# A mixture-of-experts block behind linear attention: gate logits carried with the values, and expert rows gathered through a table

## The chip, the core and the metric

The kernel runs on one core of a Trainium2 chip. The metric is the device time of one execution in microseconds (us); lower is better. The core has five engines that work side by side and meet at semaphores: TensorE (PE; its weight loads are shown apart as PEld), VectorE (DVE), ScalarE (ACT), GpSimd (POOL) and SyncE (SP), which here only issues transfers.

## What is computed

Three blocks in a row, all in float32: a decaying linear attention over 2 sequences of 768 tokens with 8 heads of 48, a mixture of 8 experts with one expert per token, and a dense block.

```python
for t in range(S):                                  # attention, per batch and head
    cur = einsum('bhd,bhe->bhde', u[None] * kt, vt)
    y[:, :, t] = einsum('bhd,bhde->bhe', rt, state + cur)
    state = w[None, :, :, None] * state + einsum('bhd,bhe->bhde', kt, vt)

logits = x @ w_gate                                 # experts: x is (1536, 384), w_gate (384, 8)
expert_idx = argmax(logits, axis=1)
gate_w = softmax(logits)[arange(N), expert_idx]
for i in range(N):                                  # tokens keep their order inside an expert
    e = expert_idx[i]
    if counts[e] < capacity:                        # capacity is 384
        disp[e, counts[e]] = x[i]; pos[i] = counts[e]; counts[e] += 1; keep[i] = True
y = einsum('ecf,efd->ecd', relu(einsum('ecd,edf->ecf', disp, w1)), w2)
out[i] = gate_w[i] * y[expert_idx[i], pos[i]]       # 0 where not kept

h = x @ w_in; g = h - tanh(h); out = g @ w_out      # dense block
```

## The kernel before

**Attention.** 12 tiles ("steps", n = 0 to 11) of 128 tokens, six per sequence, all heads at once. Inside a tile the recurrence is a product of decayed keys and queries. TensorE does, in step n and in this order: the key-query products into `pA` (lines 1140, 1144); the tile's share of the next state into `pT` (1165); the old state's share of the output into `pY` (1174), which waits until the tile before has been read out of `pY`; `own_products(n + 1)`, the diagonal term u*r*k per head (1105); `x_transposed(n - 1)`, three transposes of the finished tile (1084); once VectorE has copied the lower triangle of `pA` to `At` (880), the products of `At` with the values into `pY` (1189); `own_transposed(n + 1)` (1116); `logits(n - 1)`, three products of the transposed tile with the gate weights (1094). At n = 6, the start of the second sequence, there is no old state, and so no 1174. VectorE runs `output` (859, which makes tile x), `queries` (792), the copy to `At` (880), `keys` (784) and the new state (890) in every step. ScalarE copies transposes and logits out of PSUM and scales queries and states. GpSimd multiplies `rkf` (481), `kend` (489) and `vdiag` (507). SP loads the tiles three steps ahead (`feature_part`, `token_part`, `value_part`).

**Routing.** Tiles go in groups of 4, 4, 2 and 2 (`GROUPS`). `route1(g)` finds each token's expert on VectorE from the copied logits, a chain of some ten small dependent operations; `route2(g)` finds the gate weight, the position in the expert (from two TensorE products, `positions`) and the slot. `ROUTE1` and `ROUTE2` say in which steps they run. ScalarE scales the rows of x by the gate weight (`scale_x`; `SCALED` says when). GpSimd then scatters each tile's rows to their slots in `x_by_slot` in DRAM with an indirect DMA (`scatter`, line 472; `SENT` says when); ScalarE's queue has filled that tensor with zeros before, in nine pieces (line 650). SP loads an expert's 384 slots with a plain DMA (`expert_rows`, lines 411, 412, 421, 426). The tiles 8 to 11 are late, so for expert 0 they go to TensorE directly: `spots_of` makes a one-hot matrix and `direct` (1205) places the rows, on top of the rows that were loaded (`loaded`, 1211).

**Experts.** For expert e TensorE does `first` (72 products of 224 columns, float32 as three products of high and low parts), `transposed_rows` for expert e + 1 (1254, needs its loaded rows), and `second` (72 products). The weights are streamed by SP through four raw buffers; ScalarE makes the high part (580), VectorE the low part of w1 (849), GpSimd the low part of w2 (`low`, 460, four per expert). GpSimd's order around them is written out: four `low` of expert 0, six `token_ranks` (indirect DMAs, line 521), four `low` of expert 1, six `token_ranks`, then a loop over the other experts. A raw buffer is free for the next weights once its low part is made.

**Dense block and end.** TensorE runs without a pause; the result rows are scattered by GpSimd (550).

## Time and profile before

| | |
|---|---|
| median of 3 runs | 412.27 us (409.12 to 420.2) |
| the profiled execution: time | 410.51 us |
| its span, first to last instruction | 408.8 us |
| mean granted TensorE clock | 0.98 |
| busy: PE, PEld | 384.9 us (94%), 373.1 us (91%) |
| busy: DVE, ACT, POOL | 214.2 us (52%), 180.9 us (44%), 155.7 us (38%) |
| attention: start to the last `output` | 0 to 77.5 us |
| routing tail: to expert 0's first product | 77.5 to 92.9 us |
| experts | 92.9 to 230.6 us |
| dense block and end | 230.6 to 408.8 us |

The busy shares are means over stages that differ. TensorE is close to always busy from 92.9 us on; before that, it shares the bound with others. A line of the timeline reads: start, duration, engine, line, operation, output<-inputs, shape, count, and in brackets how long the engine was idle before and what ended that. "issue" and "remote" are idle times that nothing in the kernel's own waits explains. The clock is given as a share of 2.4 GHz.

### The profile page before, as it was taken

Reading aid. Unit: us, or ns where it says so; the run is one execution under the profiler, and the core shown is the slowest. Engines: PE = TensorE matmul, PEld = TensorE weight load, DVE = VectorE, ACT = ScalarE, POOL = GpSimd, SP = SyncE. Lnnn points to the kernel's source line nnn. Section 1 sums busy time; section 2 is a strip of 40 time slices with the busy share of each in tenths; the row PEclk is TensorE's granted clock in tenths of the full one; section 3 lists DMA queues with packets and bytes.
Section 4 is the critical chain, followed back from the end, with each engine's and each line's share of the span. In section 5 each row is a group of like instructions: output and inputs, shape, how many; then the busy total and the mean of one; then the engine's idle time right before and its main releaser. Section 6 shows DMA issues by size and latency. Waiting matters only on the chain.

```text
span 408.8 us, 10468 instructions
## 1 busy us (share of the span) xinstructions
PE 384.9 (94%) x3738; PEld 373.1 (91%) x3739; DVE 214.2 (52%) x453; ACT 180.9 (44%) x486; POOL 155.7 (38%) x132
## 2 busy tenths in 40 slices
PE   7999898698999999999999899999999999999991
PEld 7777687598999999999999899999999999999991
DVE  7667978574555655555465356615252434343340
ACT  5553456434564665756656454533022313231220
POOL 3966665435877742715517051541002000110002
PEclk9999999689999999999999999999999999999997
DMA  7989986444849478576684527000000000010001
GB/s 246 271 251 269 249 211 220 141 149 154 264 162 285 150 249 261 189 253 192 224 284 158 182 79 226 6 21 38 0 0 19 38 0 0 0 58 0 0 0 65
DMA packets 41541, 56.85 MB, mean 139 GB/s; under 512 B 3584, under 2 KB 39104, under 8 KB 41504
## 3 DMA queue, kind: packets, MB, share of 16 engines
q1 hardware_dynamic: 35936, 46.23, 36.9%
q10 hardware_dynamic: 3600, 5.31, 4.1%
q0 software_dynamic: 1968, 4.83, 3.1%
q8 instruction: 22, 0.36, 0.4%
q14 instruction: 15, 0.12, 0.1%
HBM read 46.23 MB, written 10.13 MB: 138 GB/s over the span
## 4 chain that ended last, share of the span: by engine, by line
PE 58%; issue 18%; POOL 13%; DVE 4%; DMA 2%; ACT 2%; another core or an unknown queue 1%; POOLq 0%; DVEq 0%; SPq 0%; ACTq 0%
POOL w_lo L460 11%; PE ring L1065 9%; PE ring L1067 9%; PE ring L1066 9%; PE pO L1317 8%; PE pO L1316 8%; PE pY L1189 2%; POOL token_of_rank L521 2%; PE ring L1205 2%; PE pA L1140 2%; PE pD L1094 1%; DVE At L880 1%; PE pY L1174 1%; PE pX L1084 1%
## 5 line engine op out<-in xcount | busy, mean ns | idle before, releaser
L460 POOL TENSOR_TENSOR w_lo<-raw_weights,w_hi 128x768 fp32r<-128x768 f32 x40 | 73.5, 1846 | 84.6 <-ACT w_hi L580 84.3
L1007 DVE SCALAR_TENSOR_TENSOR minus_tanh<-square,ring 128x384 f32<-128x384 f32 x64 | 35.5, 554 | 93.5 <-ACT square L730 79.1
L580 ACT ACTIVATE w_hi<-raw_weights 128x768 fp32r<-128x768 f32 x80 | 67.1, 848 | 28.5 <-DMA raw_weights<-w 28.4
L730 ACT ACTIVATE square<-ring 128x384 f32<-128x384 f32 x64 | 31.4, 491 | 94.7 <-DVE h_hi L1017 53.8
L1065 PE MATMUL ring<-yT_hi,w_hi 128*128 x192 | 65.0, 339 | 1.7 <-DVEq L1002 1.7
L1316 PE MATMUL pO<-w_hi,h_hi 128*128 128x384 f32 x192 | 64.9, 338 | 0.0
L1317 PE MATMUL pO<-w_lo,h_hi 128*128 128x384 f32 x192 | 64.8, 338 | 0.0
L1066 PE MATMUL ring<-yT_lo,w_hi 128*128 x192 | 64.8, 338 | 0.0
L1067 PE MATMUL ring<-yT_hi,w_lo 128*128 x192 | 64.8, 338 | 0.0
L1065 PE MATMUL ring<-xT_hi,w_hi 128*128 128x224 f32 x192 | 52.9, 275 | 1.6 <-issue 1.1
L849 DVE TENSOR_TENSOR w_lo<-raw_weights,w_hi 128x768 fp32r<-128x768 f32 x40 | 42.4, 1073 | 22.3 <-ACT w_hi L580 18.7
L550 POOL DMA_INDIRECT out<-out_rows,tok x12 | 11.7, 976 | 111.1 <-ACT out_rows L725 107.2
L1065 PE MATMUL pO<-h_hi,w_hi 128*128 128x224 f32 x192 | 53.2, 277 | 0.0
L1067 PE MATMUL ring<-xT_hi,w_lo 128*128 128x224 f32 x192 | 52.6, 274 | 0.6 <-issue 0.6
L1066 PE MATMUL ring<-xT_lo,w_hi 128*128 128x224 f32 x192 | 52.6, 274 | 0.0
L1067 PE MATMUL pO<-h_hi,w_lo 128*128 128x224 f32 x192 | 52.6, 274 | 0.0
L1066 PE MATMUL pO<-h_lo,w_hi 128*128 128x224 f32 x192 | 52.6, 274 | 0.0
L967 DVE SCALAR_TENSOR_TENSOR h_lo<-ring,h_hi 128x224 fp32r<-128x224 f32 x64 | 24.3, 390 | 32.9 <-ACT h_hi L697 30.9
L1065 PEld LDWEIGHTS ring<-xT_hi,w_hi 128*128 128x128 f32 x192 | 36.8, 192 | 2.8 <-issue 2.0
L1065 PEld LDWEIGHTS ring<-yT_hi,w_hi 128*128 128x128 f32 x192 | 36.0, 188 | 1.9 <-issue 1.9
L1065 PEld LDWEIGHTS pO<-h_hi,w_hi 128*128 128x128 f32 x192 | 36.8, 192 | 0.1
L1067 PEld LDWEIGHTS pO<-h_hi,w_lo 128*128 128x128 f32 x192 | 36.9, 192 | 0.0
(158 smaller groups left out, 744.1 us busy)
## 6 DMA issues: line engine op xcount, KB each, us to landing
raw_weights<-w SPq DMA_DIRECT2D x80, 384.0 KB
x_by_slot<-x ACTq DMA_DIRECT2D x9, 576.0 KB, 4.4
x_expert<-x_by_slot SPq DMA_DIRECT2D x8, 576.0 KB
kv<-kv_by_token SPq DMA_DIRECT2D x22, 192.0 KB, 4.2
rkT<-rk_by_feature SPq DMA_DIRECT2D x18, 192.0 KB, 5.1
rkT<-rk_by_feature SPq DMA_DIRECT2D x3, 512.0 KB, 4.5
x_expert<-x_by_slot SPq DMA_DIRECT2D x1, 384.0 KB
x_by_slot<-x,sloti POOLq DMA_INDIRECT x12, 4.1
```

The lines of the kernel that those rows point to most:

```text
L460: pool.tensor_tensor(lo, unit_raw(2, k), hi.bitcast(F32), ALU.subtract).then_inc(w2_ready, 1)
L550: pool.indirect_dma_start(out=out_d, out_offset=bass.IndirectOffsetOnAxis(ap=tok3[:, i:i + 1], axis=0), in_=ost[:, i, :], in_offset=None). ...
L580: act.activation(hi, unit_raw(what, k), ACT.Copy).then_inc(w1_hi if what == 1 else w2_hi, 1)
L730: act.activation(sq[:, i % 2, :], ring[i % 4][:, 0:CAP], ACT.Square, scale=THIRD ** 0.5, accum_out=sqsum[:, bass.ds(t * (2 * FC) + i, 1)]) ...
L849: dve.tensor_tensor(lo, unit_raw(1, k), hi.bitcast(F32), ALU.subtract).then_inc(w1_ready, 1)
L967: dve.scalar_tensor_tensor(out=hl[:, f, 0:cols], in0=ring[f % 4][:, 0:cols], scalar=0.0, in1=hh[:, f, 0:cols].bitcast(F32), op0=ALU.max, o ...
L1007: dve.scalar_tensor_tensor(out=nt[:, i % 2, :], in0=sq[:, i % 2, :], scalar=1.0, in1=ring[i % 4][:, 0:CAP], op0=ALU.subtract, op1=ALU.mult ...
L1065: pe.matmul(out, hi, m_hi, start=first, stop=False)
L1066: pe.matmul(out, hi, m_lo, start=False, stop=False)
L1067: return pe.matmul(out, lo, m_hi, start=False, stop=last)
L1316: pe.matmul(pO[k][:, 0:D], g, W2h[:, s, f, :], start=starts, stop=False)
L1317: last = pe.matmul(pO[k][:, 0:D], g, W2l[:, s, f, :], start=False, stop=(ends and not general))
```

## The change

- **Logits ride with the values.** A head's values get eight more columns (`DV = DH + E` = 56, tile `vg`), that hold v times the gate weights of that head. They come out of `own_products`, which now also multiplies the values by feature (a third plane of the tile `rkT`, so SP loads half as much again there) with the gate weights, and out of the transpose behind it; ScalarE copies them into `vg` (`gated_values`). All products with values or states are 56 columns wide instead of 48. The logits are then a sum over the heads of columns of x: one more `tensor_reduce` in `route1`. `x_transposed`, `xt_copy`, `logits` and `logit_copy` go.
- **Rows are stored by token.** SP stores tile n to `x_by_token` with a plain DMA once it is scaled. The zero fill and the scatters go.
- **Experts gather.** A table says which row each slot holds: `places_of` (five small VectorE operations per group, two of them new to the chain) and `spread` (two `tensor_scalar` per tile on GpSimd, 128x24 and 128x128) make one-hot tiles, `tabled` multiplies them on TensorE (8 tiles, later 4), `table_copy` reads them out on ScalarE. GpSimd then gathers an expert's three blocks of 128 rows with three indirect DMAs (`gather`), at the place in its own queue that the new loop gives.
- The parts of the routing run one or two steps earlier (`ROUTE1`, `ROUTE2`, `SCALED`); `low` for w1 of expert 0 is moved behind the routing on VectorE.

```diff
-ROUTE1 = {5: 0, 9: 1}
-ROUTE2 = {6: 0, 10: 1}
-SCALED = {8: [0, 1], 9: [2, 3], 11: [4, 5, 6, 7]}
-SENT = {9: [0, 1], 10: [2, 3], 11: [4, 5, 6, 7]}
+ROUTE1 = {4: 0, 8: 1, 10: 2}
+ROUTE2 = {5: 0, 9: 1}
+PLACES = {6: 0}
+SPREAD = {10: 0, 11: 1}
+SCALED = {6: [0], 7: [1], 8: [2], 9: [3], 10: [4, 5], 11: [6, 7]}
...
+            for n in range(STEPS):
+                sp.wait_ge(xg_ready, n + 1)
+                sp.dma_start(x_d[1 + n * P:1 + (n + 1) * P, :], row(n)).then_inc(stored[n], 16)
+            for k in range(4):
+                unit(2, 0, k)
...
+            def spread(g):
+
+                pool.wait_ge(places_ready, g + 1)
+                if g == 2:
+                    pool.wait_ge(table_full, 1)
+                first, m = GROUPS[g]
+                for n in range(first, first + m):
+                    pool.tensor_scalar(qhot[:, n % DIRECT, :], counts[:, :], reached[:, n:n + 1], None, ALU.is_equal)
+                    last = pool.tensor_scalar(phot[:, n % DIRECT, :], lanes[:, :], lane_no[:, n:n + 1], tokno[:, n:n + 1],
+                                              ALU.is_equal, ALU.mult)
+                last.then_inc(hot_ready, 1)
...
+            def expert_rows(e):
+
+                pool.tensor_copy(row3[:, :], row_i[:, e, :]).then_inc(row3_made, 1)
+                pool.wait_ge(row3_made, e)
+                for k in range(BLOCKS):
+                    gather(x_d, row3, k, xe_in)
+
+            pool.wait_ge(table_done, 1)
+            link(pool.tensor_copy(early_i[:, :], table[:, 0, 0:BLOCKS]))
+            pool.wait_ge(zero_in, 16)
+            for n in range(DIRECT):
+                pool.wait_ge(stored[n], 16)
+            gather(x_d[0:1 + DIRECT * P, :], early_i, 0, xe_in)
+            gather(x_d[0:1 + DIRECT * P, :], early_i, 1, xe_in)
+            spread(2)
+            spread(3)
+            gather(x_d[0:1 + DIRECT * P, :], early_i, 2, xe_rest_in)
+            pool.wait_ge(table_done, 2)
...
+            expert_rows(1)
...
                 for n in range(e * C, (e + 1) * C):
                     token_ranks(n)
+                pool.wait_ge(ring_full, e * RING + (RING + KD))
+                expert_rows(e + 2)
...
+            def gated_values(n):
+
+                act.wait_ge(dg_full, n + 1)
+                act.wait_ge(value_in[n % 3], 16 * (n // 3 + 1))
+                act.copy(vg[:, n % 3].rearrange("p (a b) e -> p a b e", b=2)[:, :, :, DH:DV],
...
             scale_x(10)
             scale_x(11)
+            table_copy(1)
...
+            def places_of(g, link):
+
+                first, m = GROUPS[g]
+                tiles = slice(first, first + m)
+                link(dve.tensor_tensor(allf[:, 2, tiles], allf[:, 1, tiles], limit[:, tiles], ALU.is_lt))
                 link(dve.copy_predicated(tokslot[:, tiles], allf[:, 2, tiles].bitcast(U32), allf[:, 1, tiles]))
...
+                link(dve.tensor_tensor(past[:, 0:m], bc(tokslot[:, tiles].unsqueeze(2), [P, m, Q + 1]),
+                                       bc(bounds[:, :].unsqueeze(1), [P, m, Q + 1]), ALU.is_ge))
+                link(dve.tensor_reduce(reached[:, tiles], past[:, 0:m], AX.X, ALU.add))
+                dve.scalar_tensor_tensor(out=lane_no[:, tiles], in0=reached[:, tiles], scalar=float(P),
+                                         in1=tokslot[:, tiles], op0=ALU.mult, op1=ALU.subtract).then_inc(places_ready, 1)
...
+                pe.wait_ge(feature_in[n % 3], loaded_features(n))
+                for p in range(NP):
+                    last = pe.matmul(pX[32 * p:32 * p + 2 * E + 2, D:D + P], own_gate[:, 1, p, :], rkT[:, n % 3, 2, p, :],
+                                     start=False, stop=True, skip_group_check=True)
...
+            def tabled(tiles, hot):
+
+                pe.wait_ge(hot_ready, hot)
+                for n in tiles:
+                    last = pe.matmul(pD[:, 0:Q], phot[:, n % DIRECT, :], qhot[:, n % DIRECT, :], start=(n == tiles[0]),
+                                     stop=(n == tiles[-1]))
+                last.then_inc(table_full, 1)
...
+            tabled(range(DIRECT), 2)
+            pe.wait_ge(x_ready, STEPS)
             for c in range(KD):
                 direct(8, c, near, True, False)
...
+            pe.wait_ge(table_done, 1)
+            tabled(range(DIRECT, STEPS), NG)
```

## Rows read from the trace of the kernel before

**Rows 1.** The page's slices (40 of 10.2 us): TensorE's granted clock, in tenths.

```profile
PEclk9999999689999999999999999999999999999997
```

**Rows 2.** Busy time by stretch: window, its length, PE PEld DVE ACT POOL, PEclk, DMA share, GB/s.

```profile
20.00:40.00 20.00, 18.31 (x483) 15.25 (x484) 13.12 (x20) 9.33 (x40) 12.17 (x11) 1.00 0.85 253
...
120.00:150.00 30.00, 29.77 (x267) 29.59 (x266) 17.98 (x33) 17.82 (x39) 18.36 (x13) 1.00 0.75 237
```

**Rows 3.** Chain of work that ended last, attention step 3: start, us, engine, tile, line.

```profile
25.97 0.21 PE pA L1140
...
26.99 0.60 PE pT L1165 x16
27.59 0.61 PE pY L1174 x32
28.20 0.33 PE pX L1105 x8
28.54 0.48 PE pX L1084 x3
29.01 1.07 PE pY L1189 x32
30.08 0.26 PE pX L1116
30.34 0.57 PE pD L1094 x6
30.91 0.21 PE pA L1140
```

**Rows 4.** Timeline: one 128x128 operation of GpSimd, three rows of VectorE around `route1(0)`.

```profile
1.88 0.29 POOL L444 TENSOR_SCALAR_AFFINE_SELECT before<-ones 128x128 f32<-128x128 f32 x1
...
39.49 1.07 DVE L800 TENSOR_TENSOR ldiff<-logit,lmax 128x32 f32<-128x32 f32 x1
...
41.77 0.19 DVE L808 TENSOR_TENSOR onehot<-prio,allf 128x32 f32<-128x32 f32 x1
...
43.04 0.56 DVE L859 TENSOR_TENSOR x<-vdiag,pY 128x384 f32<-128x384 f32 x1
```

**Rows 5.** Timeline, all engines: two stalls, the routing tail, expert 0's first product.

```profile
62.90 0.48 ACT L584 COPY xT<-pX 128x384 f32<-128x384 f32 x1 [3.03 <-remote]
...
77.48 0.55 DVE L859 TENSOR_TENSOR x<-vdiag,pY 128x384 f32<-128x384 f32 x1 [2.03 <-remote]
...
80.93 4.08 PE L1205 MATMUL ring<-kw,x 128*128 128x224 f32 x10
...
86.69 1.48 PE L1211 MATMUL ring<-ident,x_expert 128*128 128x128 f32 x12
...
88.00 2.46 PE L1205 MATMUL ring<-At,x 128*128 128x224 f32 x12
...
92.94 0.36 PE L1065 MATMUL ring<-xT_hi,w_hi 128*128 128x224 f32 x1 [1.14 <-issue]
```

**Rows 6.** Timeline of GpSimd and TensorE in the first experts.

```profile
105.16 1.52 POOL L521 DMA_INDIRECT token_of_rank<-tokrow,rank_i  x1
...
112.39 0.96 POOL L521 DMA_INDIRECT token_of_rank<-tokrow,rank_i  x1 [0.30 <-issue]
115.67 7.26 POOL L460 TENSOR_TENSOR w_lo<-raw_weights,w_hi 128x768 fp32r<-128x768 f32 x4 [2.32 <-ACT w_hi L580]
...
119.20 0.82 PE L1254 MATMUL ring<-ident,x_expert 128*128 128x128 f32 x6
...
136.43 0.82 PE L1254 MATMUL ring<-ident,x_expert 128*128 128x128 f32 x6
```

**Rows 7.** The page's DMA issues: out<-in, queue, count, KB each, median us to landing.

```profile
rkT<-rk_by_feature SPq DMA_DIRECT2D x3, 512.0 KB, 4.5
x_by_slot<-x,sloti POOLq DMA_INDIRECT x12, 4.1
...
out<-out_rows,tok POOLq DMA_INDIRECT x12, 2.5
```

340 lines of the change are left out of this document (161 added, 179 removed).

## The prediction

> **What bounds the kernel now.** I read the page's slices first, then the busy times by stretch, the chain of waits, and the timeline of single stretches. TensorE runs at its upper level, 2.4 GHz, in all but two slices of 10.2 us, around 71 to 92 us [rows 1]. From the first expert on it is the bound: 29.77 us busy of 30 [rows 2]. Between 20 and 40 us it is busy for 18.31 of 20 us, and the transfer engines take a share of 0.85 at 253 GB/s [rows 2]. One attention step of the chain, 4.94 us from `pA` to `pA`, has TensorE work alone in it: `pA` 1.02 (25.97 to 26.99), then 0.60, 0.61, 0.33, 0.48, 1.07, 0.26 and 0.57 [rows 3]. So a product less in a plain step is time less. This isn't so where the router runs: `route1(0)` holds VectorE from the end of its state copy to the `output` at 43.04, nearly 4 us, because some of its operations last 1.07 instead of 0.19 us beside GpSimd's [rows 4]. The routing tail, from the `output` at 77.48 to expert 0's first product at 92.94, is 15.46 us of waiting in turns [rows 5]. So the change acts at three places: the steps, the tail, and GpSimd's queue in the experts, where it adds.
>
> **Attention, part by part.** All terms are us against the profiled execution.
> - Start: the first feature load grows from 512 to 768 KB. A load of 512 KB lands after 4.5 us [rows 7], and 262 kB at 253 GB/s [rows 2] are 1.0 us; part of it hides behind the powers that VectorE makes meanwhile. Bounds 0 and +1.0, taken +0.8.
> - A plain step loses the transposes (0.48) and the logits (0.57) and gains a second set of own products (0.33) [rows 3]: -0.72. The three groups that become 56 wide (0.60 + 0.61 + 1.07 = 2.28 us) cost nothing if their count sets them, and 2.28 x 8/48 = 0.38 if the columns do. Half, +0.2, since four small products overlap in the array. So -0.5 per step, and 11 x -0.5 = -5.5 if all steps were plain. VectorE's 13.12 us and GpSimd's 12.17 us of 20 [rows 2] cover a step of 4.4 us.
> - The new copy `gated_values` goes to ScalarE behind the transpose, and `pT` waits for it. `pA` (1.02) lies between [rows 3]; the copy is a few tenths. Nothing, but 0.3 per step if ScalarE is late by that much more. Behind it in ScalarE's queue stand the diagonals, for which GpSimd's `vdiag` waits, a step ahead of need.
> - `route1(0)` moves from step 5 to 4, `route1(1)` from 9 to 8. At step 5 it stood ahead of step 6, which has no old-state products; now 1174 of the next step needs the `output` that is queued behind it. It keeps its nearly 4 us and gets a reduce of 256 elements, about 0.3 (the ones of 32 elements take 0.19 [rows 4]). TensorE has about 1.8 us of other work meanwhile (`pA`, `pT`), and the rest of 4.3 us, less the tail of the step before, is waited for: I take +1.2 for each, +2.4 together, bounds 0 and +4.
> - `places_of` is five operations, of 0.19 to 0.3 us, for each of the first two groups, less three that `route2` loses: +0.6 each, +1.2.
> - The scatters held GpSimd, and two idle times are there that no wait of the kernel explains, 3.03 us on ScalarE before 62.90 and 2.03 us on VectorE before 77.48 [rows 5]. Both stand where scatters are issued, but also where the program runs into new code. About 3 us of the last steps hang on them; the nearest bounds are 0 and -3 and nothing separates them, so -1.2.
> - The zero fill (9 x 576 KB) goes, and 3 x 64 KB of features and 32 KB of values are more per step: fewer bytes, no term.
>
> Sum to the last `output`: 0.8 - 5.5 + 2.4 + 1.2 - 1.2 = -2.3, so near 75.2.
>
> **Tail.** The logits of the last tile come 2.8 us sooner after its `output`, as neither transposes nor copies nor products precede `route1(3)`. What ends last is then another path: 16 passes of `tabled` at 0.1 us (the pace of line 1211's 12 in 1.48, less at full clock [rows 5]) 1.6; copies 0.7; the first gather's issue 1.3; the second landing 4.1 after its issue [rows 7]; `loaded` 1.5 [rows 5]; the second `tabled` 0.8; `table_copy`, which now stands in front of the splits in ScalarE's queue, 0.3, and the splits 1.1; and TensorE's restart 1.4. That is 12.8 at the upper clock. The stretch from 80.93 shows 0.41 per product at 1.2 GHz against 0.2 from 88.00 on [rows 5]; with all TensorE parts doubled it is 12.8 + 1.6 + 1.5 + 0.8 = 16.7, and 18 with `direct` late too. `spread` (two operations per tile, 0.15 and 0.29 by [rows 4]; 0.9 a pair if two scalars slow it) hides behind the last step for tiles 0 to 7, and behind the gathers for 8 to 11. I take 15.0: -0.5. Expert 0 starts at 92.94 - 2.3 - 0.5 = 90.1.
>
> **Experts.** SP's plain loads become GpSimd's. An indirect issue takes 112.39 + 0.96 - 105.16 = 8.2 us for six, or 1.37 each [rows 6]; three are 4.1 us, and the last lands 2.5 to 4.1 us after its issue began [rows 7], 1.5 to 3.1 behind its end. GpSimd's queue from expert 0's first product on: expert 1's gathers until +4.6, four `low` 7.3 [rows 6], six ranks 8.2, expert 2's gathers 4.1: done at +24.2, landed at +25.7 to +27.3. TensorE wants these rows at 119.20 - 92.94 = +26.3 [rows 5, 6]: a stall of 0 to 1.0. Then 7.3 + 8.2 + 4.1 more: done at +43.8, landed at +45.3 to +46.9; wanted at 136.43 - 92.94 = +43.5 [rows 5, 6]. Both stalls together are 1.8 to 3.4; as single issues take 1.52 [rows 6], I take 3.2. From expert 3 on the queue holds 7.3 + 4.1 = 11.4 of 16.7 us, and the gathers hide. Queued behind them is `low`, for which `second` waits, then SP's next raw weights; `low` of expert 1 ends some 1.7 us later against TensorE than now, which the raw buffers cover.
>
> The Trainium skill ("DMA: Bandwidth & Descriptors", Anatomy of one DMA — SWDGE (gpsimd) path) gives a GpSimd transfer 2.0 us plus its bytes over 436 GB/s, so 2.45 us for 192 KB. The trace agrees for the result rows (2.5) and not for the slot rows (4.1) [rows 7]; by the page the stalls would be 1.8, at the lower end. The same page (SWDGE vs HWDGE vs iDMA) speaks against the change: descriptors that GpSimd writes can be held up by VectorE, and those of SP can't.
>
> Sum: -2.3 - 0.5 + 3.2 = +0.4 on 410.5, so 410.9. The profiled execution lies 1.8 under the median of the runs; I say 411.0. About 2% (8.2 us) is what a measurement of this kernel can tell from no change: 404.0 and 420.5.
>
> **Rivals.**
> - *The gains come whole.* The unexplained idle times go with the scatters (-1.8 more), the tail runs at the upper clock (12.8: -2.2 more), the gathers land after 2.5 us (-1.4). Then 405.5; with plain steps where I put `route1` (-2.4) 403. For it: the clock fell only around 75 us, after idle times; against it: `tabled` waits for GpSimd and leaves TensorE idle as well.
> - *GpSimd becomes the bound (the other side).* VectorE holds up each gather's descriptors. The price is three gathers in each of two experts in a row: with 2 us each instead of 1.37, 2 x 1.9 = +3.8, so 414.7. It passes 420.5 at 1.37 + 9.5/6 = 3 us each, or where the landings are long too. For it: issues of 0.96 and of 1.52 us side by side, and operations of VectorE that stretch to 1.07 beside GpSimd's [rows 4, 6]; against it: none of the 12 issues was near 2 us.
> - *The tail stays at 1.2 GHz throughout*, 18 us: +3.0, 413.9. For it: so it is now, for two slices [rows 1].
> - *The steps don't get shorter*, as VectorE or the larger feature loads set them: +3 to +5, 414 to 416. Against it: 1.0 MB per step in 4.4 us is 230 GB/s, under the 253 reached [rows 2].
>
> **Chances.** Forecast, 407 to 415: 0.50. Gains whole, 402 to 407: 0.22, two thirds of it under 404. Slow tail or steps that stay, 413 to 418: 0.13. GpSimd the bound, 414 to 424: 0.15, most of it over 418. So faster 0.17, the same 0.68, slower 0.15, and a range of 403.5 to 419.0.
>
> **What the profile would show.** Plain steps of 4.4 us from `pA` to `pA`, steps 5 and 9 longer by over 1 us with TensorE waiting for `output`; the last `output` near 75; expert 0's first product near 90; TensorE waiting for the gathers at experts 1 and 2, and nowhere later; GpSimd without a gap there. The forecast is wrong if TensorE never waits for a gather, if one costs 2 us or more, or if the clock stays up through the tail.

## The result, and the profile after

The changed kernel takes 428.5 us (median of 4 runs, 428.2 to 428.6) where the kernel before takes 411.5 on the same chip: a ratio of 1.043, with an interval of 1.038 to 1.048. It is slower. The forecast was 411.0, with slower at 0.15. The profiled execution took 428.6, its span is 426.8 us against 408.8. Some executions of a kernel last 1 to 3% longer than its others, at a lower granted clock (one of the kernel before took 420.2 us), and the ratios here and below leave them out.

Three places carry the 18 us of the span. The table gives, in us from the span's start, the places by which the prediction counted.

| | before | forecast | after | against the forecast |
|---|---|---|---|---|
| last attention `output` starts | 77.48 | 75.2 | 82.40 | +7.2 |
| tail, from there to expert 0's first product | 15.46 | 15.0 | 20.74 | +5.7 |
| expert 0's first product | 92.94 | 90.1 | 103.14 | |
| transposed rows of expert 3 begin | 136.43 | | 154.52 | |
| from the first product to there | 43.49 | 46.7 | 51.38 | +4.7 |
| the dense part's first product | 230.64 | | 249.13 | |

From expert 3 on nothing more is lost: 154.52 - 136.43 is 18.1, and 249.13 - 230.64 is 18.5. TensorE's granted clock by slices of 10.7 us, to be read against [rows 1], is under 0.9 in five slices ahead of the last one, where it was in two:

```profile
PEclk9989699759998999999999999999999999999997
```

Busy time by stretch, with the columns of [rows 2]. Between 20 and 40 us TensorE is busy for 16.82 us instead of 18.31, at a mean clock of 0.91, and gets less far. Fewer bytes flow (168 GB/s, not 253), at nearly the same share of the transfer engines (0.83). Between 120 and 150 us TensorE is no longer full and GpSimd is busy 24.50 of 30 us:

```profile
20.00:40.00 20.00, 16.82 (x460) 13.70 (x452) 13.91 (x23) 8.37 (x37) 11.75 (x10) 0.91 0.83 168
120.00:150.00 30.00, 25.77 (x216) 25.37 (x215) 14.18 (x27) 15.44 (x34) 24.50 (x22) 0.94 0.60 180
```

The view of the transfer queues for the same 20 us (20 to 40) says more than the mean rate: packets, MB, and the share of the 16 engines' time. The kernel before, where q1 holds SP's loads and q10 the zero fill:

```profile
q1 hardware_dynamic: 1423, 2.70, 48.2%
q10 hardware_dynamic: 1554, 2.31, 35.9%
```

The kernel after:

```profile
q1 hardware_dynamic: 1303, 3.30, 81.1%
```

So nearly half of the 253 GB/s was the zero fill. SP's loads alone grew from 2.70 to 3.30 MB, and the engines' time for them from 48.2% to 81.1%.

**An undisturbed step** is what the forecast said, or a little better. TensorE's timeline, one step from `pA` to `pA` (29.39 to 33.53), which answers [rows 3]: 4.14 us, where it was 4.94 and 4.4 was forecast. It follows a stop, in which the other engines could get ahead; in the run without the third plane (below) such steps take 4.4 to 4.5. The transposes of `x` and the logits are gone, L1152 is new, and the groups that became 56 wide took 0.61, 0.62 and 1.07 from start to start, as before: the count sets them, not the columns.

```profile
29.39 0.33 PE L1194 MATMUL pA<-rw,kw 64*64 64x128 f32 x2
...
30.41 0.68 PE L1222 MATMUL pT<-v_and_gate,kend 128*64 128x56 f32 x16
31.02 0.69 PE L1231 MATMUL pY<-st,rw 64*64 64x56 f32 x32
31.64 0.41 PE L1148 MATMUL pX<-rkf,own_gate 128*18 128x128 f32 x8
31.87 0.40 PE L1152 MATMUL pX<-rkvT,own_gate 128*18 128x128 f32 x8
32.20 1.15 PE L1242 MATMUL pY<-v_and_gate,At 128*64 128x56 f32 x32
33.27 0.33 PE L1162 MATMUL pX<-ident,own_by_head 128*128 128x128 f32 x1
33.53 0.33 PE L1194 MATMUL pA<-rw,kw 64*64 64x128 f32 x2
```

**But few steps are undisturbed.** Inside `pY` TensorE stands still with nothing to wait for that the profile shows ("issue"): 4.7 us in five places, the longest ahead of 25.62, where the kernel before has 2.7 in six, none over 0.84. The longest of the kernel before, then that of the changed kernel:

```profile
22.94 0.33 PE L1174 MATMUL pY<-st,rw 64*64 64x48 f32 x7 [0.84 <-issue]
...
25.62 0.90 PE L1231 MATMUL pY<-st,rw 64*64 64x56 f32 x23 [2.21 <-issue]
```

After this stop the granted clock was 0.50 between 26 and 28 us; after the wait for the `output` at step 5 (2.4 us, and 0.70 of "issue" behind it) it was 0.50 to 0.67 between 42 and 50.

**The tail** (timeline, all engines, answers [rows 5]). First GpSimd makes one-hot tiles: 0.33 and 0.79 us for each, 1.12 together where the forecast had 0.44. TensorE waits 2.12 us for `At`, which stands on VectorE behind `places_of(1)`, and 1.78 for the last one-hot; from 80 to 96 us its clock is 0.50. The table's first product takes 3.61 us (1.6 was forecast), then ScalarE, which has waited 9.13 us for it, makes the copy, and only behind that copy come the scaled rows 8 and 9 for which `direct` at 88.56 waits:

```profile
77.37 0.79 POOL L502 TENSOR_SCALAR lane_hot<-lanes,lane_number,token_number 128x128 f32<-128x128 f32 x1
...
80.33 1.96 PE L1242 MATMUL pY<-v_and_gate,At 128*64 128x56 f32 x32 [2.12 <-DVE At L940]
...
82.40 0.62 DVE L917 TENSOR_TENSOR x<-vdiag,pY 128x448 f32<-128x448 f32 x1 [1.34 <-PE pY L1242]
...
84.07 3.61 PE L1177 MATMUL pD<-quarter_hot,lane_hot 128*128 128x24 f32 x16 [1.78 <-POOL lane_hot L502]
...
87.72 0.18 ACT L685 COPY table<-pD 128x24 f32<-128x24 f32 x1 [9.13 <-PE pD L1177]
...
87.80 1.12 ACT L671 ACTIVATE x<-x,gate 128x384 f32<-128x384 f32 x2
...
88.56 2.58 PE L1252 MATMUL ring<-kw,x 128*128 128x224 f32 x6 [0.87 <-ACT x L671]
...
98.89 1.47 PE L1258 MATMUL ring<-ident,x_expert 128*128 128x128 f32 x12
...
103.14 0.36 PE L1124 MATMUL ring<-xT_hi,w_hi 128*128 128x224 f32 x1 [0.51 <-DVE xT_lo L996]
```

**The first experts** (GpSimd's timeline, answers [rows 6]). A gather costs what one of the rank scatters costs, 0.96 and a gap of 0.30. The queue starts late, since the copy of the row numbers at 105.12 waited 3.11 us for TensorE, and another 0.8 us passes between each such copy and the first gather that reads it. The six rank scatters took 9.5 us here (8.2 in [rows 6]).

```profile
105.12 0.18 POOL L539 COPY row<-row_of_slot 128x3 int32<-128x3 int32 x1 [3.11 <-PE ring L1126]
106.11 0.99 POOL L533 DMA_INDIRECT x_expert<-x_by_token,row  x1 [0.81 <-POOL row L539]
...
109.62 7.20 POOL L475 TENSOR_TENSOR w_lo<-raw_weights,w_hi 128x768 fp32r<-128x768 f32 x4
117.00 1.54 POOL L568 DMA_INDIRECT token_of_rank<-tokrow,rank_i  x1 [0.17 <-issue]
...
126.46 0.20 POOL L539 COPY row<-row_of_slot 128x3 int32<-128x3 int32 x1
...
130.06 0.95 POOL L533 DMA_INDIRECT x_expert<-x_by_token,row  x1 [0.30 <-issue]
131.04 7.11 POOL L475 TENSOR_TENSOR w_lo<-raw_weights,w_hi 128x768 fp32r<-128x768 f32 x4
```

TensorE waits for these rows at experts 2 and 3 (the two waits that the prediction places at experts 1 and 2 of its count):

```profile
134.13 1.08 PE L1304 MATMUL ring<-ident,x_expert 128*128 128x128 f32 x6 [4.24 <-DMA x_expert<-x_by_token,row]
...
154.52 0.87 PE L1304 MATMUL ring<-ident,x_expert 128*128 128x128 f32 x6 [1.73 <-DMA x_expert<-x_by_token,row]
```

The waits are 6.0 of the 7.9 us that the experts lose. A part of the rest is the clock: between 134 and 138 us, behind the longer wait, it was 0.58.

The page's DMA issues, with the columns of [rows 7]: the first three feature loads land after 7.0 us (4.5 before), and the keys by token, 192 KB as before, after 6.9 (4.2 before).

```profile
rkvT<-rkv_by_feature SPq DMA_DIRECT2D x3, 768.0 KB, 7.0
...
k_tok<-k_by_token SPq DMA_DIRECT2D x10, 192.0 KB, 6.9
x_expert<-x_by_token,row POOLq DMA_INDIRECT x24, 4.8
```

### The profile page after: what moved, and what is told of

Read it like the earlier page. It is cut to its first block, busy times and chain, and to the rows that moved or that the text cites. A ratio compares the mean times of both kernels' runs of the same rounds, so it can differ in the third digit from the quotient of the medians.

```text
span 426.8 us, 10564 instructions
## 1 busy us (share of the span) xinstructions
PE 386.3 (91%) x3754; PEld 373.1 (87%) x3755; DVE 222.4 (52%) x465; ACT 177.9 (42%) x476; POOL 195.6 (46%) x187
## 4 chain that ended last, share of the span: by engine, by line
PE 76%; POOL 7%; DVE 7%; issue 4%; DMA 2%; ACT 1%; DVEq 0%; ACTq 0%; POOLq 0%; SPq 0%
PE ring L1124 12%; PE ring L1126 12%; PE ring L1125 12%; PE pO L1366 8%; PE pO L1367 8%; PE pO L1124 5%; PE pO L1126 4%; PE pO L1125 4%; PE ring L1252 2%; POOL token_of_rank L568 2%; POOL w_lo L475 2%; PE pY L1242 2%; POOL lane_hot L502 1%; PE ring L1304 1%; PE pA L1194 1%
## 5 line engine op out<-in xcount | busy, mean ns | idle before, releaser
L907 DVE TENSOR_TENSOR w_lo<-raw_weights,w_hi 128x768 fp32r<-128x768 f32 x40 | 43.3, 1095 | 21.7 <-ACT w_hi L641 21.0
L1125 PEld LDWEIGHTS pO<-h_lo,w_hi 128*128 128x128 f32 x192 | 37.6, 196 | 0.0
```

Of the source, the lines that this page charges most:

```text
L907: dve.tensor_tensor(lo, unit_raw(1, k), hi.bitcast(F32), ALU.subtract).then_inc(w1_ready, 1)
L1125: pe.matmul(out, hi, m_lo, start=False, stop=False)
```

## Experiments: the experts

All runs stand against the kernel before, run in between on the same chip. "After" is the changed kernel, 428.5 us.

**Gathers ahead of the rank scatters.**

```diff
+                pool.wait_ge(ring_full, e * RING + (RING + KD))
+                expert_rows(e + 2)
                 if e == 0:
                     pool.wait_ge(rank_ready, 1)
                 for n in range(e * C, (e + 1) * C):
                     token_ranks(n)
-                pool.wait_ge(ring_full, e * RING + (RING + KD))
-                expert_rows(e + 2)
```

> The changed kernel, but GpSimd issues expert e + 2's three gathers before the six token_ranks of expert e = 0 and 1 instead of behind them. Theory 'order': the 8.3 us that the experts of the changed kernel lose between expert 0's first product (103.1) and the dense block (249.1, 18.5 behind before, against 10.2 at the first product) are GpSimd's queue, the gathers standing behind the ranks. TensorE then no longer waits 4.24 and 1.73 us for x_expert, and the time falls by about 7 us, from 428.5 to 421 to 422. Theory 'price': a gather is slow in itself (4.8 us to landing, while VectorE and the weight loads run), wherever it stands: the waits stay, and the time falls by 0 to 2 us.

Measured 428.5 (ratio 1.032, 1.022 to 1.043): no gain. The theory of the order failed in its time and the rival in its waits. The waits for gathered rows are gone, but expert 3 still starts 21.2 us behind expert 2 (151.81 and 130.58). TensorE now waits for what comes through the splits. GpSimd, from one set of splits to the next:

```profile
130.73 7.19 POOL L475 TENSOR_TENSOR w_lo<-raw_weights,w_hi 128x768 fp32r<-128x768 f32 x4
137.87 0.91 POOL L539 COPY row<-row_of_slot 128x3 int32<-128x3 int32 x1
139.60 1.00 POOL L533 DMA_INDIRECT x_expert<-x_by_token,row  x1 [0.82 <-POOL row L539]
...
151.08 7.22 POOL L475 TENSOR_TENSOR w_lo<-raw_weights,w_hi 128x768 fp32r<-128x768 f32 x4
```

There is no idle time in it beyond the gaps between issues. 151.08 - 130.73 is 20.4 us of splits, copy, gathers and ranks, and 16.7 us is what an expert costs TensorE. The order within the queue brings little where the sum is too long: from expert 0's first product to the dense part's first, this run takes 143.9 us, the changed kernel 146.0, the kernel before 137.7, and the 2 us are lost again elsewhere.

**The rank scatters behind the splits of the last four weight sets.**

```diff
-                for n in range(e * C, (e + 1) * C):
-                    token_ranks(n)
 ...
             for e in range(E - 2, E + 2):
                 for k in range(4):
                     low(e, k, e % 2)
+                for n in range((e - E + 2) * 3, (e - E + 3) * 3):
+                    token_ranks(n)
```

> The changed kernel with the twelve token-rank scatters taken out of experts 0 and 1 and put behind the split halves of the last four weight sets (three each), where GpSimd waits for weights anyway; nothing is left out. Theory 'sum on the queue': in the changed kernel expert 0 to 1 takes 21.4 us and 1 to 2 20.4 us where an expert costs 16.7, because GpSimd has 7.2 us of splits, 9.5 us of rank scatters and some 4.5 us of row copy and gathers, 21.2 us in all; without the 9.5 us the experts follow each other at 16.9, 17.0 and 16.8 us, the dense part starts some 8 us earlier (241 instead of 249.1) and the time is 420.5 (419 to 422). Rival 'price of a gather' (each gather lands 4.8 us after its issue whatever stands before it, and TensorE waits for it): the waits at experts 1 and 2 stay at 2 us or more each and the time is 425 or more. Rival 'moved, not saved': the scatters hold back the second layer's last splits, and part of the 8 us comes back between 235 and 260 us.

Measured 425.5 (ratio 1.025). The experts follow each other at 17.0, 16.9, 16.7 and 16.8 us, as the theory of the sum says, up to 214.20; then one takes 20.4. ScalarE stood still there, for nothing that the profile names, at a place where its program branches.

```profile
225.03 0.59 ACT L758 CAST yT_hi<-pO 128x224 f32 x2 [3.59 <-remote]
```

So 3.8 us of the 8 came through here. In the three later runs with the same edit (below) this stop is absent. In the one with one-pass transpositions every expert keeps 16.7 to 16.8 us, and from expert 0's first product to the dense part's first it takes 137.1 us, the kernel before 137.7; in the other two a single expert takes 18.3 and 17.8. So GpSimd's sum is the loss in the experts, nearly all of it. What makes ScalarE stop in some programs is open: no packet of an instruction queue (they are explained below) lies within such a stop or in the 3 us ahead of it, here or in the two runs with the changed kernel further down that have one.

## Experiments: the attention steps

**The router's moves undone.**

```diff
-ROUTE1 = {4: 0, 8: 1, 10: 2}
-ROUTE2 = {5: 0, 9: 1}
-PLACES = {6: 0}
-SCALED = {6: [0], 7: [1], 8: [2], 9: [3], 10: [4, 5], 11: [6, 7]}
+ROUTE1 = {5: 0, 8: 1, 10: 2}
+ROUTE2 = {6: 0, 9: 1}
+PLACES = {7: 0}
+SCALED = {7: [0], 8: [1], 9: [2, 3], 10: [4, 5], 11: [6, 7]}
```

> The changed kernel, but the routing of tiles 0 to 3 one step later, as before: route1(0) in step 5, route2(0) in step 6, places_of(0) in step 7, and the scaling of tiles 0 and 1 one step later. Theory 'placement': at step 4 route1(0) stands ahead of a step that needs the output queued behind it (TensorE waits 2.38 us before pY of step 5, and its clock then falls to half for some 7 us), at step 5 it doesn't: 3 to 4 us less, 425. Rival: the routing costs VectorE the same wherever it stands, and the later steps take over the wait: within 1 us of 428.5.

Measured 429.0 (ratio 1.033), as the rival said. The wait for the `output` at step 5 goes, and 4 us of "issue" inside `pY` stand in its place; the last `output` starts at 82.15 instead of 82.40.

```profile
42.45 0.89 PE L1231 MATMUL pY<-st,rw 64*64 64x56 f32 x19 [4.02 <-issue]
```

The move, which the forecast priced at +2.4, shows no cost here, but only since this stop covers it. In the run without the third plane (below) the stop is absent, and TensorE waits 2.4 us for the `output` at step 5 there.

**The logits alone.** The kernel before, and of the change only the 56 columns, the third plane and the new own products; scatters, zero fill and slot loads as before.

```diff
-        rkT = sb("rkT", [P, 3, 2, NP, P], F32, att)
+        rkT = sb("rkvT", [P, 3, 3, NP, P], F32, att)
 ...
-                    x_transposed(n - 1)
 ...
+                for p in range(NP):
+                    last = pe.matmul(pX[32 * p:32 * p + 2 * E + 2, D:D + P], own_gate[:, 1, p, :], rkT[:, n % 3, 2, p, :],
+                                     start=False, stop=True, skip_group_check=True)
```

> The kernel before, with one part of the change alone: the logits ride with the values (features, gated_values, 56 columns, the reduce in route1), while scatter by slot, zero fill, SP's loads of expert rows and the steps of the routing stay as before. Theory 'gain in the steps': plain steps fall from 4.94 to 4.15 us as in the changed kernel, the start is 1.3 us later, the tail loses transposes and logits (2.8 us): 405 to 409 against 411.4. Rival: the larger feature loads stretch the code stalls inside pY (2.21 us in one step of the changed kernel, with its clock fall), so that the steps give nothing: 410 to 414.

Measured 415.8 (ratio 1.010, 1.005 to 1.016). This half of the change was to bring 5.5 us. Its last `output` starts at 85.77, 8.3 later than before, and TensorE stands still 9.6 us inside `pY`:

```profile
46.96 0.56 PE L1160 MATMUL pY<-st,rw 64*64 64x56 f32 x19 [3.74 <-issue]
```

Its tail is 14.5 us, one less than before. TensorE's program differs from both others here, which by itself can move the attention's end by some us (see the run with the program moved, below), so the 8.3 us aren't the loads' alone.

**The load alone.** The kernel before, with a third plane that is loaded and not read.

```diff
-        rkT = sb("rkT", [P, 3, 2, NP, P], F32, att)
+        rkT = sb("rkT", [P, 3, 3, NP, P], F32, att)
 ...
-        "rk_by_feature": np.stack([by_feature(r), by_feature(k)], axis=2),
+        "rk_by_feature": np.stack([by_feature(r), by_feature(k), by_feature(v)], axis=2),
```

> The kernel before with one thing more: each feature load brings a third plane (the values by feature), which nothing reads: 768 KB instead of 512 KB for the first three steps, 288 KB instead of 192 KB for each half later. Theory 'the loads': the larger loads alone make TensorE stand still in the attention steps (issue time inside the key-value products of pY, 9.6 us in five stalls with the logits alone, 2.0 us before) and bring its clock to half there; the last attention output then starts 3 to 8 us later than 77.5 and the time is 415 to 419. Rival 'the products': it is the added products and the widened operands that cost the time; the last output stays within 1.5 us of 77.5 and the time at 412 to 413.5. The first A product starts 1.3 us later under the first, as in the changed kernel.

Measured 425.4 against 414.2 (ratio 1.024, 1.017 to 1.031): with bytes that nobody reads the kernel takes some 10 us longer. Where they go isn't shown. The profile is of an execution of 433.6 us, where the other four took 424.0 to 425.9, and it has ScalarE standing still as in the run with the rank scatters late, 3.56 us ahead of 91.83 and 3.24 ahead of 145.62, the latter in the experts, where no feature is loaded. The logits alone carry the same loads at 415.8, so the 10 us aren't the price of the bytes in the attention. That is read from the next run.

**The third plane not loaded.** The changed kernel, whose logit products read the keys in place of the values.

```diff
-        rkT = sb("rkvT", [P, 3, 3, NP, P], F32, att)
+        rkT = sb("rkT", [P, 3, 2, NP, P], F32, att)
 ...
-                    last = pe.matmul(pX[32 * p:32 * p + 2 * E + 2, D:D + P], own_gate[:, 1, p, :], rkT[:, n % 3, 2, p, :],
+                    last = pe.matmul(pX[32 * p:32 * p + 2 * E + 2, D:D + P], own_gate[:, 1, p, :], rkT[:, n % 3, 1, p, :],
```

> The changed kernel without the third plane of the feature load: the products that make the gate logits read the keys by feature, which are there anyway, in place of the values by feature. So the logits, the routing and the output are not the reference's; the instructions of all engines are the same in number and size, and 2.4 MB less flow in the attention steps. Theory 'the loads' (the feature load of 288 KB a half instead of 192 KB, and 768 instead of 512 KB at first, is what TensorE's instruction fetch and the first step wait behind): the start wins back 1.3 us, the standing still inside pY falls from 4.7 to about 2 us, the clock drops of 26 to 30 us and 42 to 50 us go or shrink, the last output comes at 77 to 79.5 instead of 82.4 and the time is 423.5 to 426. Rival 'instructions': the stalls lie where TensorE's program reaches the end of what has been fetched, whatever flows; nothing but the start moves and the last output comes at 81 or later.

Measured 421.9 (ratio 1.030, 1.018 to 1.042), 1.6 us below what the theory gave, and the rival is out. The last `output` starts at 74.07, 8.3 us before that of the changed kernel and 3.4 before that of the kernel before; both theories had placed it later. TensorE's instructions are the same in number and order as in the changed kernel, so what is gained is the loads' doing. The clock is full from 20 to 40 us, and VectorE gets through 18.49 us of work where it got through 13.91:

```profile
20.00:40.00 20.00, 16.94 (x496) 13.92 (x494) 18.49 (x33) 8.78 (x41) 14.14 (x13) 1.00 0.65 159
```

The longest "issue" time inside `pY` is 0.35. The remaining loads land sooner too:

```profile
rkT<-rkv_by_feature SPq DMA_DIRECT2D x18, 192.0 KB, 3.8
...
k_tok<-k_by_token SPq DMA_DIRECT2D x10, 192.0 KB, 3.9
```

So the shorter steps were there, and the third plane's loads took them and 4.9 us more. All of it reaches the end of the profiled execution: the span is 418.4 instead of 426.8 (the medians of the runs differ by 6.6). The waits for gathered rows stay (2.42 us at expert 2, 0.83 at expert 3), and the tail is longer than in the changed kernel, 22.9 us, with a stop that isn't there in the changed kernel:

```profile
96.99 0.55 PE L1124 MATMUL ring<-xT_hi,w_hi 128*128 128x224 f32 x1 [3.72 <-issue]
```

From there to the dense part's first product this run takes 2.1 us less than the changed kernel, which makes up for it.

**The third plane in a load of its own, behind the keys by token.**

```diff
-                        sp.dma_start(rkT[rows, n % 3], by_feature_d[n, rows]).then_inc(feature_in[n % 3], 16)
+                        sp.dma_start(rkT[rows, n % 3, 0:2], by_feature_d[n, rows, 0:2]).then_inc(feature_in[n % 3], 16)
 ...
+                        sp.dma_start(rkT[rows, n % 3, 2], by_feature_d[n, rows, 2]).then_inc(vfeature_in[n % 3], 16)
```

> The changed kernel with the third plane of the feature load (the values by feature) taken out of that load and loaded by itself behind the keys by token, with a semaphore of its own; same bytes, nothing is left out. Theory 'the loads': what VectorE and GpSimd need first lands as early as before the change (5.1 us instead of 7.0 us after its issue), the start wins back 1.0 to 1.3 us, but the same bytes still flow, so TensorE's stalls inside pY stay (3 us or more in all) and the last output stays near 81 to 82; the time is 426.5 to 428. Rival 'size of the first load': only the late landing counts, the stalls shrink to the 2.0 us of the kernel before and the last output comes at 79 or earlier, the time at 425 or below.

Measured 430.5 (ratio 1.037). The last `output` starts at 79.57, between the two expectations, so the size of the first load may be part of it, but nothing is left at the end: ScalarE stands still for 5.2 us in expert 1, again at a branch and without a reason in the profile.

**What TensorE stands still for.** The profile has a transfer queue of its own kind, "instruction". Read in windows of a quarter of a microsecond, it shows where each 16 KB transfer of queue q8 starts. For the changed kernel, in the window 22.75 to 23.00 (packets, MB, share of 16 engines):

```profile
q8 instruction: 1, 0.02, 31.4%
```

2.9 us behind it TensorE goes on, at 25.62. It is so for nearly every stop:

| kernel | TensorE goes on at (idle before) | transfer started in the window from |
|---|---|---|
| before | 22.94 (0.84), 33.20 (0.30), 38.41 (0.55), 67.06 (0.33) | 19.75, 30.50, 35.25, 64.50 |
| after | 19.02 (0.76), 25.62 (2.21), 35.83 (0.41), 42.96 (0.70), 73.32 (0.64) | 16.25, 22.75, 32.75, 40.00, 71.00 |
| logits alone | 20.77 (2.68), 33.67 (1.67), 46.96 (3.74), 59.38 (1.29) | 18.00, 31.00, 43.75, 56.00 |
| no third plane | 30.39 (0.35), 96.99 (3.72) | 27.50, 94.25 |

The distance is 2.3 to 3.4 us throughout. Three small stops of the kernel before (0.33 to 0.39, around 62 and 74 us) have none at that distance, and most transfers have no stop behind them: the changed kernel has twelve up to its last `output` and five stops. To test it, TensorE's program was moved against its steps, with sixteen small products of zeros ahead of the first step, in time in which it was idle:

```diff
             keep_warm(14, zero, pR[:, 0:P])
+            for _ in range(16):
+                pe.matmul(pR[0:8, 0:8], zero[:, 0:8], zero[:, 0:8], start=True, stop=True)
```

> The changed kernel with sixteen more products of 8 x 8 zeros behind TensorE's first warm-up (some 64 instructions with their weight loads), done before the first A product may start; same loads, nothing is left out. What is behind it: in the runs so far a 16 KB transfer of the instruction queue starts 2.3 to 3.4 us ahead of nearly every place where TensorE stands still with nothing to wait for. Theory 'instruction fetch': TensorE's program is moved by a quarter of such a piece against the steps, so the transfers start at other places of the steps, and the stalls (0.76 us at 19.0, 2.21 at 25.6, 0.41 at 35.8, 0.70 at 43.0, 0.64 at 73.3 inside pY) change place and size, again 2.3 to 3.4 us behind a transfer's start; the time may move 3 us either way. Rival 'data or the engine itself': the stalls stay at the same steps inside pY with the same sizes within 0.3 us, and so does the time (428.5).

Measured 426.2. All stops inside `pY` are gone, and there are stops inside `pA` and `pT`: 28.32 and 38.31 below, 62.99 (1.30) and 69.68 (1.46). The transfers started from 25.25, 35.25, 60.00 and 67.25: 3.1, 3.1, 3.0 and 2.4 us ahead.

```profile
28.32 0.27 PE L1200 MATMUL pA<-rw,kw 64*64 64x64 f32 x1 [2.70 <-issue]
...
38.31 0.27 PE L1200 MATMUL pA<-rw,kw 64*64 64x64 f32 x1 [1.06 <-issue]
```

The loads are the same, and the stops moved with the program: TensorE stands still for its own instructions. The last `output` starts at 78.40, 4.0 us sooner, by idle instructions alone. That isn't one kernel's scatter: three programs with the same attention (the changed kernel, the gathers ahead, the rank scatters late) start it between 81.73 and 82.84. Nor is it less standing still, which adds up to 6.5 us here and to 4.7 there: the clock stays full behind the stop of 2.70, where it fell to 0.50 behind the 2.21 of the changed kernel. What a stop costs depends on where it falls.

Since the distance from the transfer to the restart is the same without the third plane (2.9), what the loads delay must lie ahead of the transfer's start. The records don't show when a transfer is asked for, so that part is inferred.

The Trainium skill ("Runtime: NRT & Kernel Launch", Instruction fetch mechanics) has the 16 KB blocks and the queue of each engine, and says that crossing a block's end is "mostly hidden". By that rule the stops would be worth next to nothing; here they were up to 4.0 us each. Many of the long ones fall where the transfer engines are full (a share of 1.01 between 24 and 26 us in the changed kernel, of 1.02 between 44 and 47 with the logits alone), but the 3.72 us of the run without the third plane don't (0.33 between 94 and 97 us), so full engines aren't the only condition.

## Experiments: the tail, and all together

**TensorE kept busy.** Products of ones into a free bank ahead of its longest waits: 10 at step 5, 6 at step 9, 8 ahead of the last `At`, 6 ahead of the first table.

```diff
+                if n in WARM:
+                    keep_warm(WARM[n], ones[:, :], pD[:, 0:P])
                 if n > 0:
                     pe.wait_ge(x_ready, n)
```

> The changed kernel, with products of ones into an unused PSUM tile where TensorE waits: 10 before pY of step 5, 6 before pY of step 9, 8 before At's products of step 11, 6 before the first tabled. They leave the result alone. Theory 'clock': TensorE's clock stands at half from 42 to 49 us and from 80 to 97 us since it idled just before; filled waits keep it at full, and the half-clock work there (about 9 us of 18 busy) is saved: 5 to 8 us less, 421 to 423. Rival: the clock falls anyway, or the tail is set by waits for other engines and not by TensorE's pace: 427 to 429, and up to 1 us more where the filling is late.

Measured 426.0 (ratio 1.027), between theory and rival. The first product comes at 98.62 instead of 103.14, with a tail of 18.7, and the dense part's first at 244.73 instead of 249.13; from there to the end it takes 1.8 us longer than the changed kernel, and why isn't shown. As the products are also instructions that move the program, the last `output`, at 79.94, may owe its gain to either.

**The one-hot tiles on VectorE, the table's copy behind rows 8 and 9.** GpSimd keeps those of tiles 0 to 3, one a step; VectorE makes the other eight.

```diff
-SPREAD = {10: 0, 11: 1}
+SPREAD = {7: [0], 8: [1], 9: [2], 10: [3]}
 ...
+                    dve.tensor_scalar(phot[:, n % DIRECT, :], lanes[:, :], lane_no[:, n:n + 1], tokno[:, n:n + 1],
+                                      ALU.is_equal, ALU.mult).then_inc(hot_ready, 1)
 ...
-            table_copy(0)
             scale_x(8)
             scale_x(9)
+            table_copy(0)
             expo(3)
```

> The changed kernel with the one-hot tiles made elsewhere: those of group 0 still on GpSimd, but one tile a step from step 7 on, those of groups 1 to 3 on VectorE (0.15 to 0.3 us each by its other instructions of that size, instead of 1.1 us a tile on GpSimd), and ScalarE's copy of the first table behind the scaling of rows 8 and 9 instead of ahead of it. Nothing is left out. Theory 'the tail waits for GpSimd and for the copy': the second table no longer waits for its one-hots and rows 8 and 9 are scaled 5 us earlier, the stretch from the last output to the first expert product falls from 20.7 us to 16 to 18 and the time to 424 to 426. Rival 'the copy and the gathers set it': the gathers of expert 0 start no earlier (their table is copied later), the stretch stays at 20 or grows, and the time stays at 428. Rival 'VectorE': 16 more instructions on VectorE around the last output move it back by 1 to 2 us and eat the gain.

Measured 429.9 (ratio 1.039). The tail falls to 18.7 us, a little short of the 16 to 18 of the theory. ScalarE stands still twice in the experts, 3.2 and 3.3 us, and the end shows nothing of it.

**The third plane replaced by transpositions.** TensorE transposes the values, already loaded by token, a step ahead, and ScalarE copies them out.

```diff
+            def values_transposed(n):
+                pe.wait_ge(value_in[n % 3], 16 * (n // 3 + 1))
+                for p in range(NP):
+                    last = pe.matmul(pD[0:DV + DH, p * P:(p + 1) * P],
+                                     vg[:, n % 3].rearrange("p h e -> p (h e)")[:, 2 * p * DV:2 * p * DV + DV + DH], ident[:, :],
+                                     start=True, stop=True, skip_group_check=True)
+                last.then_inc(vt_full, 1)
```

> The kernel before with the logits riding along with the values, and nothing else of the change, as in the run with the logits alone (last output 85.8, first product 14.5 us behind it, 415.8 us); but the values by feature aren't loaded: TensorE transposes the loaded values a step ahead (four products of 104 columns into a bank that is free) and ScalarE copies them out (one copy of 104 x 512). Nothing is left out. Theory 'the loads': without the third plane the shorter step comes through at last: it was to save 0.5 us a step by my sum, the last output comes at 73 to 77.5, the first product 14.5 us behind it, and the time is 404 to 409. Rival 'longer programs': four more products a step bring TensorE's standing still back, and ScalarE's copy of 0.6 us stands in the way of the decayed queries; the last output comes at 80 or later and the time is 411 or more.

Measured 419.4 (ratio 1.020, 0.999 to 1.041). The rival was right: the stops inside `pY` are gone, but three stand in `pA` and `pX` (0.99, 0.49 and 1.79 us), a plain step is 5 to 6 us, and the last `output` starts at 87.30, 1.5 us behind that of the logits alone.

In the changed kernel, together with the edits of the warm, rank and tail runs:

> The changed kernel with all remedies together: values transposed on TensorE in place of the third plane, the rank scatters behind the splits of the last four weight sets, TensorE kept warm ahead of its longest waits, the one-hot tiles of groups 1 to 3 on VectorE, and the table's first copy behind the scaling of rows 8 and 9. Nothing is left out. If the four causes are separate and their sizes add, the 428.5 us fall by 3 to 6 (loads), 3.8 to 8 (ranks), 2 (warm) and 2 (tail): 409 to 417, with the last output at 77 to 80, the first product 17 to 18.7 us behind it and the experts following each other at 16.8 us. If they hide each other (the gathers wait for the tables, whatever the rest does) it is 418 or more.

Measured 417.3 (ratio 1.021, 1.008 to 1.033), just above what was expected of separate causes. The clock is full from the start to 130 us, the experts follow each other at 16.8 us but for one of 18.3, and the tail is 14.4 us, a microsecond less than before the change. TensorE's timeline in this tail: the table's product takes 1.86 us, not 3.61, and `direct` follows it at once.

```profile
82.13 1.86 PE L1203 MATMUL pD<-quarter_hot,lane_hot 128*128 128x24 f32 x16
83.84 1.38 PE L1285 MATMUL ring<-kw,x 128*128 128x224 f32 x6
...
95.62 0.37 PE L1141 MATMUL ring<-xT_hi,w_hi 128*128 128x224 f32 x1 [0.49 <-DVE xT_lo L1013]
```

What is left is the attention: 5.2 us a step, with TensorE full, the transposing products 1.12 of it.

```diff
-                    last = pe.matmul(pD[0:DV + DH, p * P:(p + 1) * P],
+                    last = pe.transpose(pD[0:DV + DH, p * P:(p + 1) * P],
```

> The kernel with all remedies again, but the four products that transpose the values are issued as transpositions, as the kernel before issues its own (one instruction for 128 x 128 there, two for a plain product): in the run with all remedies these eight instructions took 1.12 us of a step in which TensorE had no idle time (5.1 to 5.2 us a step). Nothing is left out. Theory 'TensorE is the bound of the step with transposed values': four instructions in some 0.5 us shorten the step to 4.5 to 4.7 us, the last output comes at 75 to 77 instead of 81.2, the tail stays at 14.4 us and the experts at 16.8 us each, and the time is 406 to 411, at or below the kernel before. Rival 'the chain over VectorE and ScalarE (At, then own rows, then the diagonal) is right behind': the step stays at 4.9 us or more, the last output at 79 or later and the time at 412 to 416.

Measured 414.9 (ratio 1.013, 1.007 to 1.019). The four now take 0.65, but the step is 5.0: TensorE waits for ScalarE's copy, which stands behind the decayed queries.

```profile
52.50 0.41 PE L1178 MATMUL pX<-vT,own_gate 104*18 104x128 f32 x8 [0.70 <-ACT vT L642]
```

The rival was right. So the transpositions go ahead of the carried state's products, and the copy ahead of the decayed queries:

```diff
                 if n + 1 < STEPS:
-                    decayed_queries(n + 1)
                     vt_copy(n + 1)
+                    decayed_queries(n + 1)
```

> The run with one-pass transpositions once more, with the transpositions of the next values right behind the A products, ahead of the carried state's products, and ScalarE's copy of them ahead of the decayed queries: in that run TensorE waited 0.3 to 1.1 us a step for that copy (8.4 us with the weight loads' share), which stood behind the decayed queries while ScalarE had been idle 1.3 to 1.7 us before them. Nothing is left out. Theory 'the copy is late': the wait goes, a step takes 4.5 to 4.7 us instead of 5.0, the last output comes at 74 to 77 instead of 78.9 and the time is 409 to 412.5 (against 414.9, the kernel before 411.8). Rival 'TensorE's own sum': its instructions of a step add up to 5.2 us with their overlaps, the step stays at 4.9 or more and the time at 413.5 or more.

Measured 413.1 over 12 runs against 412.1 over 17 (ratio 1.0065, 1.002 to 1.011). This lies between theory and rival. A plain step is 4.7 us and the last `output` starts at 77.17. The tail stays long: in the profiled execution, one of 416.0 us, it takes 19.1 us, 3.99 of them a wait for expert 0's gathered rows. As it stands this is the change with the remedies for every loss that was found: 15 us better than as it was made, within 1% of the kernel before, and not faster than it. No version that beats both was found.

## Why the prediction was wrong, point by point

- **Plain steps, -0.5 each.** Right: 4.14 us for the one undisturbed step of the changed kernel, and 4.4 to 4.5 in the run without the third plane, against the 4.4 forecast. The 56 columns cost nothing, so the half of 0.38 taken for them was too much. The reading that VectorE covers such a step is right with nothing to spare: it was busy 18.49 of 20 us in that run.
- **"Fewer bytes, no term."** This is the step that failed first and most. It counted bytes over the whole attention and found fewer. The third plane's loads cost 8.3 us (82.40 against 74.07). Of these the start is 1.3 and the stops inside `pY` 4.4 (4.72 against 0.35); the rest isn't split, but the clock between 20 and 40 us was 0.91 against 1.00, and the other loads landed later. The size holds for this place of the program against the steps: with the program moved, the same loads leave the last `output` at 78.40, 4.3 above. That the loads hold back TensorE's instructions on the engines that both share is the inference, as said above. The rival named larger feature loads, with +3 to +5, and dismissed them by a mean rate, 230 GB/s under the 253 reached. Nearly half of those 253 was the zero fill, and what flowed after the change was 168 GB/s at a share of 0.83, so the rate was no measure of how full the engines were.
- **Start, +0.8.** The first `pA` starts at 9.07 instead of 7.80: +1.3. Without the third plane it starts at 7.82, so it is the same cause.
- **The rest of the attention sum.** Less the start's 0.8, the sum came to 74.4 for the last `output`; without the third plane it is 74.07. That the sum fits is in part luck. From one `output` to the next, the steps that hold `route1` of the first two groups take 7.60 and 7.20 us in that run, against 7.43 and 7.23 before, while a plain step falls from 4.94 to some 4.45. So against a plain step they grew by 0.7 and 0.5, where +2.4 was taken for the moves and +1.2 for `places_of`, and other steps gained less than the plain ones.
- **Tail, 15.0.** The 12.8 at the upper clock was a fair sum (14.4 in the run with all remedies). The step that failed here is the choice of the clock and of what hides `spread`. GpSimd took 1.12 us for a tile, not 0.44 (the 0.9 was named and set aside), TensorE stood still for it and for `At`, and its clock was at half from 80 to 96 us; the table's copy held rows 8 and 9 behind it on ScalarE, which the sum didn't have at all. Even the bound for a slow clock, 18, was too low.
- **Experts, +3.2.** The mechanism was right, both waits are where they were forecast, and the size was off: 8. On GpSimd's queue the copy's wait for TensorE (some 2 us), the 0.8 between copy and gather, and the ranks (9.5 instead of 8.2) were missing. A gather in these two experts wasn't dearer than forecast (1.26 with its gap, 1.37 taken), and the longest of all took 1.70, so the rival's 2 us each didn't come. What decides is that 20.4 to 21.4 us of GpSimd's work stand against 16.7 of TensorE's. The rival's name fits, GpSimd as the bound; its reason, VectorE holding up the descriptors, doesn't.
- **A gather's landing.** It was within the 2.5 to 4.1 taken where it counted: the last rows of experts 2 and 3 landed 3.9 and 3.8 us after their issue began. The median of all 24 is 4.8, as those of the later experts, for which nobody waits, took 4.6 to 6.9. The Trainium skill ("DMA: Bandwidth & Descriptors", Anatomy of one DMA — SWDGE (gpsimd) path) would have 2.45 us for 192 KB, an estimate by its formula; no gather of this trace landed in less than 3.1.
- **The scatters' stalls, -1.2.** Not tested by a run of its own. ScalarE and VectorE have no such stop over 1.5 us in the attention and the tail of the changed kernel, but neither have they with the logits alone, which keeps the scatters. So the scatters by themselves don't make them, and the term is open.

## What to carry to other kernels

Price a larger load by what shares its engines at that moment, the engines' own instructions among them; a mean rate over the stage says nothing. If an engine stands still with "issue" in the middle of a long unrolled group, look for a transfer of the instruction queue some 3 us ahead of it, before you look for a data wait. Between two programs whose instructions differ, a few us may be the place of these transfers alone; a run that changes only the data, as the one without the third plane, is free of that. Where work moves to an engine's queue, add up everything that the queue holds in one round and compare with the round of the bounding engine; order helps little when the sum is too long.

## What was not expected of the hardware

- TensorE's stops for instructions were 0.3 to 4.0 us long, nearly each with a 16 KB transfer starting 2.3 to 3.4 us ahead of its end, and they moved with the program when some instructions were put in front. A shift that does no work changed the last `output` by 4 us: differences of 1% between two versions of such a kernel may be nothing but that.
- A 128x128 operation of GpSimd with two scalars by pointer took 0.79 us (up to 1.31), where another kind without them took 0.29 [rows 4]. On VectorE the same operation took 0.34 to 0.43 in the run with all remedies.
- The transfer engines were as full at 168 GB/s (a share of 0.83) after the change as at 253 (0.85) before it [rows 2]. SP's loads alone took 48.2% of the engines' time for 2.70 MB before, 81.1% for 3.30 MB after and 62.5% for 3.10 MB without the third plane. Why isn't shown.
- ScalarE stood still for 3.2 to 5.2 us in the experts in four of the programs (the rank scatters late, the load alone, the third plane by itself, the tail), in three of them where its program loops and branches. The kernel before has stops of 3.03 us ahead of 62.90 [rows 5] and 3.71 ahead of 78.26, in unrolled code; the changed kernel has none. The cause is open.
